# A reordered front with a third mask tile, and a sync queue that holds three loads for another one

## The chip, the cores and the metric

The program runs on one core of one Trainium2 chip. The metric is the device time of one execution in microseconds (us); lower is better. The core has a matrix engine (TensorE, PE in the profile, with its weight loads as PEld), a vector engine (DVE), a scalar engine (ACT), a general engine (GpSimd, POOL) and a sync engine (SP) that here only issues transfers. ACT and POOL issue a few transfers too. Rows ending in q (SPq, ACTq, POOLq) are the issuing side of such a transfer.

## What is computed

Two batches of 8 heads, 768 positions, head size 40: a gated recurrent attention, computed in chunks of 128 positions, then two feed-forward layers of width 1536 over the resulting 1536 x 320 matrix.

```python
for t in range(S):                                   # per batch and head
    m_new = max(f[t] + m, i[t])                      # stabiliser
    C = exp(f[t] + m - m_new) * C + exp(i[t] - m_new) * outer(v[t], k[t])
    n = exp(f[t] + m - m_new) * n + exp(i[t] - m_new) * k[t]
    y[t] = sigmoid(o[t]) * (C @ q[t]) / max(abs(n @ q[t]), 1)
x = (sigmoid(x @ w_gate) * (x @ w_val)) @ w_out      # first layer
x = ((x @ w_a) * (x @ w_b)) @ w2_out                 # second layer
```

## The kernel before

Every (batch, position block) pair is a chunk n, 12 in all; n % 2 is the batch. The first four chunks (0 to 3) are done alone, in a stretch called the front here. It ends when the first product of the feed-forward layer, `up(0, 0)` (line 580), starts. From there on TensorE runs `up` and `down` (line 597) units without a break, and the work of the chunks 4 to 11 is put between them. The order of each engine's work is written out by hand.

In a chunk, TensorE does four things. `spread` (line 440) multiplies a selection matrix with a tile `arow` (128 x 1024): its rows are a triangular mask except for rows 0 and 32, which receive the high and the low half of a running maximum (`a_hi`, `a_lo`) by transfers; the product lays that row out over 128 partitions, in PSUM. `scores` (line 477) multiplies keys `k` and queries `q_blk`, in two halves; a half needs both. `values` takes the state times scaled queries `q` (line 493; only from chunk 2 on) and then adds the weights `pt` times values `vk` (line 502). `to_state` (line 516) adds to the state and needs `v_w`. `turn` (line 528) transposes the finished rows, and `columns` (line 537) the gates.

ACT makes `pt` (`weigh`, line 687) from the spread rows; DVE multiplies it with the scores (`product`, line 893), zeroes one row of it (`dve_fix`, line 896), and divides the values (`combine`, lines 903 to 911). POOL weighs the values (`weigh_v`, 1099), multiplies with the output gate (`open_x`, 1109 and 1110), and scales the queries (`scale_q`, 1117), for which `load_scaled` on SP brings a copy of the queries (`q`, line 328) and a scale row repeated over 40 partitions (`i_rep`, line 333, three transfers). That scale row was made by ACT (`i_rows`, line 737) and goes through a scratch tensor in HBM (`i_scratch`, line 350).

Chunks use two sets of tiles in turn, so `arow[0]` serves the chunks 0, 2 and 4: the rows of chunk 2 are loaded only when `spread(0)` has read the tile (`pe_ab`). The keys and queries of chunk 3 come from POOL's own transfer queue (lines 1183 and 1186), with a semaphore of their own, `ld_q_own`, complete at 64. The other loads of the front go out from SP in written order, and a wait there holds everything behind it. Two layers' weights come as 24 tiles `w_raw` (line 346), split into `w_hi` and `w_lo`.

Of the kernel before, what the change touches and what calls it, by code (L numbers as in the profile page):

```python
# [19 lines left out]
F32 = mybir.dt.float32  # L20
# [7 lines left out]
P = 128  # L28
# [3 lines left out]
VW = HD + 1  # L32
# [32 lines left out]
def use_of(n):  # L65

    return n // 2 if n < ALONE else n - 2

# [23 lines left out]
def build(nc, f_in, i_in, q_in, kq3_in, vk_in, o_in, w1_in, w2_in, consts_in, bm_in, out):  # L92
    ctx = ExitStack()
    with ctx:
# [49 lines left out]
        both = [sb("k_both", [TRI, HEADS * P]), q_blk[0]]  # L144
        stack = [sb(f"{x}_stack", [TRI, HEADS * P], F32R) for x in "kq"]
# [35 lines left out]
        pool_q, pool_v, pool_d, pool_x = (sem(n) for n in ("pool_q", "pool_v", "pool_d", "pool_x"))  # L181
        ld_q_own, pool_wup = sem("ld_q_own"), sem("pool_wup")
# [88 lines left out]

        @block.sync
        def _(sp):
            def load_rows(n):

                s = set_of(n)
                if n > ALONE:
                    sp.wait_ge(act_e, 2 * n)
                else:
                    wait(sp, pe_ab, 2 * before(n) + 2)  # L280
                if n > ALONE:
                    sp.dma_start(levels[s][:, :],
                                 a_dram[n * HEADS * P:(n + 1) * HEADS * P].partition_broadcast(P)).then_inc(ld_a[s], 16)
                    return
                for at, tile in ((HI, a_hi), (LO, a_lo))[:1 if n < BATCH else 2]:
                    sp.dma_start(arow[s][at:at + 1, :].bitcast(F32), row_source(tile, n)).then_inc(ld_a[s], 16)  # L286
# [7 lines left out]
            def load_q(n):  # L294

                s = set_of(n)
                if n >= BATCH:
                    load_k(n)
                for j, k in ((0, 3), (1, 3), (2, 2)):
# [54 lines left out]
            load_k(0)  # L354
            load_k(1)
            sp.wait_ge(dve_zero, 1)
            load_q(0)
# [9 lines left out]
            load_v(1)  # L367
            sp.wait_ge(dve_split, 4)
# [60 lines left out]
        def _(pe):  # L429
            def spread(n):  # L430

                s = set_of(n)
                pe.wait_ge(ld_a[s], 32 * (use_of(n) + 1))
                for half in range(2):
                    if n < BATCH:
                        pass
                    else:
                        pe.wait_ge(act_e, (0, 4, 6)[n - 2] + half + 1)
                        wait(pe, act_cols, 4 if n == 2 and half == 0 else 0)
                    pe.matmul(spread_bank(n, half)[:, :], sel[:, :], arow[s][:, half * HALF:(half + 1) * HALF],  # L440
                              start=True, stop=True).then_inc(pe_ab, 1)
# [37 lines left out]

            def values(n):  # L480
# [15 lines left out]
                if n <= ALONE:  # L496
                    pe.wait_ge(dve_fix, n + 1)
# [108 lines left out]
            scores(0, 0)  # L606
            pe.wait_ge(ld_ident, 16)
# [66 lines left out]
        def _(act):  # L674
# [78 lines left out]
            def rows_out(group):  # L753

                for tb in (0, 2):
# [8 lines left out]
                    else:  # L764
# [12 lines left out]
                     tri_t[:, :].unsqueeze(1).to_broadcast([P, HEADS, P])).then_inc(tri_set1, 1)  # L777
            act.wait_ge(dve_split, 2)
# [15 lines left out]
            for c in range(2, CHUNKS):  # L794
                i_rows(c)
# [5 lines left out]
            x_high(0)  # L801
            x_high(1)
# [47 lines left out]
        def _(dve):  # L850
# [34 lines left out]
            def product(n, half):  # L885
# [8 lines left out]
                if half and n <= ALONE:  # L894
                    dve.wait_ge(dve_p, 2 * n + 2)
                    dve.memset(pt[s][LO:LO + 1, LO - 1::P], 0.0).then_inc(dve_fix, 1)
# [96 lines left out]
            dve.memset(q_blk[0][:, :], 0.0).then_inc(dve_zero, 1)  # L993
# [99 lines left out]
        def _(pool):  # L1093
# [34 lines left out]
            def mask(n):  # L1128

                level = levels[set_of(n)][:, :].rearrange("s (h t) -> s h t", t=P)  # L1130
                pool.wait_ge(ld_a[set_of(n)], 32 * (BATCH + 1) + 16 * (n - ALONE))
# [24 lines left out]
            for at in (HI, LO):  # L1156
# [12 lines left out]
                               channel_multiplier=-1).then_inc(pool_own, 1)  # L1169
            pool.wait_ge(act_cols, 2)  # L1170
            weigh_v(0)
            weigh_v(1)
# [9 lines left out]
            pool.wait_ge(pe_s, 4)  # L1182
            pool.dma_start(k3[1][:, :], kq3_in[3, :, 0:3 * P]).then_inc(ld_q_own, 16)
            for j, k in ((0, 3), (1, 3), (2, 2)):
                own = slice(j * HD, (j + 1) * HD)
                pool.dma_start(q_blk[1][own, 3 * j * P:(3 * j + k) * P],
                               kq3_in[3, own, 3 * P:(3 + k) * P]).then_inc(ld_q_own, 16)
# [85 lines left out]
```

## Time and profile before

| | us |
|---|---|
| median of 3 runs (lowest, highest) | 465.87 (465.13, 466.97) |
| the profiled execution, its own time | 466.42 |
| its span, first to last instruction | 464.7 |
| TensorE busy in the span | 457.4 |
| first `up` product starts | 35.02 |

The profiled execution's time is 1.7 us more than its span. The span is counted from the first instruction, and all positions below are us from there. After 35 us the chain that ended last consists of TensorE's units `up` and `down` and chunk work between them, one behind the other.

### The profile page before, as it was taken

How to read it: one execution, taken by the hardware profiler on the slowest of the kernel's cores; microseconds unless marked ns; L12 is line 12 of the kernel's file. 1: busy time of each engine (PE TensorE's matmuls, PEld its weight loads, DVE VectorE, ACT ScalarE, POOL GpSimd, SP SyncE). 2: the span in 40 equal slices, each digit the busy share in tenths (PEclk: the TensorE clock that was granted, in tenths of full speed). 3: DMA queues.
4: the chain of work that ended last, by engine and by line, in shares of the span. 5: the costliest groups of instructions: out<-in, count | busy, mean ns of one | idle time of the engine just before them, and what ended most of it. 6: DMA issues, size and time to landing. Idle time of an engine off the chain costs nothing.

```text
span 464.7 us, 6645 instructions
## 1 busy us (share of the span) xinstructions
PE 457.4 (98%) x2527; PEld 404.6 (87%) x2527; DVE 206.4 (44%) x365; ACT 197.2 (42%) x362; POOL 87.7 (19%) x99
## 2 busy tenths in 40 slices
PE   8989999999999999999999999999999999999996
PEld 5888899898889899888889889889988998898896
DVE  8858876766564644434132253222313222322322
ACT  5954949567382846234253352213222221312222
POOL 4573322303313020102454360000000000000000
PEclk9989999999999999999999999999999999999999
DMA  5878595542524460001322300000000000100001
GB/s 157 233 214 300 162 271 189 161 161 85 161 84 126 117 225 10 1 1 31 112 98 63 130 0 1 1 1 0 26 31 1 1 1 0 58 0 1 0 1 57
DMA packets 22005, 38.06 MB, mean 82 GB/s; under 512 B 2910, under 2 KB 16225, under 8 KB 21973
## 3 DMA queue, kind: packets, MB, share of 16 engines
q1 hardware_dynamic: 21605, 36.58, 25.7%
q10 hardware_dynamic: 208, 0.71, 0.5%
q8 instruction: 20, 0.33, 0.3%
q0 software_dynamic: 160, 0.35, 0.2%
q14 instruction: 12, 0.10, 0.1%
HBM read 35.55 MB, written 2.04 MB: 81 GB/s over the span
## 4 chain that ended last, share of the span: by engine, by line
PE 94%; DMA 2%; SPq 1%; POOL 1%; issue 1%; DVE 0%; POOLq 0%; DVEq 0%
PE bank L580 57%; PE bank L597 27%; PE bank L502 3%; PE bank L468 1%; PE bank L493 1%; PE bank L516 1%; PE bank L558 1%; PE bank L528 1%; DMA vk<-vk_in 1%; SPq L286 1%; DMA f_row<-f_in 1%; DMA i_scratch<-f_row 0%; PE bank L477 0%; POOL q L1117 0%; DMA arow<-a_lo 0%
## 5 line engine op out<-in xcount | busy, mean ns | idle before, releaser
L751 ACT CAST h_hi<-h_ff 128x512 fp32r<-128x512 f32 x72 | 44.6, 619 | 175.5 <-PE bank L597 95.2
L580 PE MATMUL bank<-xt,w_hi 128*128 128x512 f32 x360 | 117.9, 392 | 0.0
L968 DVE TENSOR_TENSOR h_lo<-h_ff,h_hi 128x512 fp32r<-128x512 f32 x72 | 52.8, 733 | 122.4 <-ACT h_hi L751 122.4
L962 DVE TENSOR_TENSOR h_ff<-bank,s_ff 128x512 f32<-128x512 f32 x72 | 49.8, 691 | 110.0 <-PE bank L580 106.0
L580 PE MATMUL bank<-xt,w_lo 128*128 128x512 f32 x216 | 84.3, 390 | 0.0
L580 PEld LDWEIGHTS bank<-xt,w_hi 128*128 128x128 f32 x360 | 66.2, 188 | 12.8 <-issue 0.2
L744 ACT ACTIVATE s_ff<-bank 128x512 f32<-128x512 f32 x72 | 43.0, 597 | 75.0 <-PE bank L580 74.1
L580 PE MATMUL bank<-xt,w_hi_end 128*128 128x512 f32 x180 | 58.8, 392 | 0.0
L580 PE MATMUL bank<-xt,w_hi_mid 128*128 128x512 f32 x180 | 58.8, 391 | 0.0
L580 PEld LDWEIGHTS bank<-xt,w_lo 128*128 128x128 f32 x216 | 40.5, 188 | 8.7
L597 PE MATMUL bank<-w_hi,h_hi 128*128 128x320 f32 x144 | 45.0, 313 | 0.0
L597 PE MATMUL bank<-w_lo,h_hi 128*128 128x320 f32 x144 | 44.4, 309 | 0.0
L597 PE MATMUL bank<-w_hi,h_lo 128*128 128x320 f32 x144 | 44.4, 308 | 0.0
L580 PE MATMUL bank<-xt,w_lo_end 128*128 128x512 f32 x108 | 42.2, 390 | 0.0
L580 PE MATMUL bank<-xt,w_lo_mid 128*128 128x512 f32 x108 | 42.2, 390 | 0.0
L580 PEld LDWEIGHTS bank<-xt,w_hi_mid 128*128 128x128 f32 x180 | 33.3, 188 | 6.4
L580 PEld LDWEIGHTS bank<-xt,w_hi_end 128*128 128x128 f32 x180 | 33.3, 188 | 6.4
L597 PEld LDWEIGHTS bank<-w_lo,h_hi 128*128 128x128 f32 x144 | 27.1, 188 | 0.7
L597 PEld LDWEIGHTS bank<-w_hi,h_hi 128*128 128x128 f32 x144 | 27.0, 188 | 0.6
L597 PEld LDWEIGHTS bank<-w_hi,h_lo 128*128 128x128 f32 x144 | 27.0, 188 | 0.0
L1139 POOL TENSOR_TENSOR w_lo<-w_raw,w_hi 128x1088 fp32r<-128x1088 f32 (+1 forms) x7 | 16.9, 2419 | 41.7 <-ACT w_hi L723 41.7
L580 PEld LDWEIGHTS bank<-xt,w_lo_end 128*128 128x128 f32 x108 | 20.3, 188 | 4.3
(128 smaller groups left out, 685.3 us busy)
## 6 DMA issues: line engine op xcount, KB each, us to landing
w_raw<-w_in SPq DMA_DIRECT2D x24, 544.0 KB, 4.0
vk<-vk_in SPq DMA_DIRECT2D x12, 344.0 KB, 3.2
levels<-a_scratch SPq DMA_DIRECT2D x7, 512.0 KB
k_both<-kq_in SPq DMA_DIRECT2D x21, 120.0 KB
q_blk<-kq_in SPq DMA_DIRECT2D x21, 120.0 KB
y<-rows_t SPq DMA_DIRECT2D x12, 160.0 KB, 1.9
q<-kq_in SPq DMA_DIRECT2D x10, 180.0 KB
osig_b<-o_in SPq DMA_DIRECT2D x8, 160.0 KB, 2.5
```

The source lines that it names most:

```text
L286: sp.dma_start(arow[s][at:at + 1, :].bitcast(F32), row_source(tile, n)).then_inc(ld_a[s], 16)
L468: mm = pe.matmul(st[:, h * P:(h + 1) * P], stack[0][:, own], stack[1][:, own], start=True, stop=True)
L493: mm = pe.matmul(acc[:, h * VW:(h + k) * VW], q3[s][:, x * P:(x + 1) * P], cst[p][:, h * VW:(h + k) * VW], start=(x == 0), stop=False)
L502: mm = pe.matmul(acc[:, h * VW:(h + 1) * VW], pt[s][:, h * P:(h + 1) * P], vk[s][:, h * VW:(h + 1) * VW], start=(n < BATCH and h == 0), st ...
L516: mm = pe.matmul(sc[0:TRI, h * VW:(h + k) * VW], vk[s][:, row:row + TRI], v_w[n % 2][:, h * VW:(h + k) * VW], start=True, stop=True)
L580: mm = pe.matmul(up_bank(u, gv)[:, :], w_part(low, f, (gv * 3 + kt) * P, P), xt[:, xb * TOK + g * TG:xb * TOK + (g + 1) * TG], start=(j == ...
L597: mm = pe.matmul(OB[tb][:, 0:DM], h[r][:, tb * P:(tb + 1) * P], w_part(low, f, W1C, DM), start=(f == 0 and j == 0), stop=(f == NF - 1 and ...
L744: act.activation(s_ff[u % 2][:, :], up_bank(u, 0)[:, :], ACT.Sigmoid if u < UNITS // 2 else ACT.Copy).then_inc(act_s, 1)
L751: act.copy(h_hi[u % 2][:, :], h_ff[u % 2][:, :]).then_inc(act_h, 1)
L962: dve.tensor_tensor(h_ff[u % 2][:, :], up_bank(u, 1)[:, :], s_ff[u % 2][:, :], ALU.mult).then_inc(dve_h, 1)
L968: dve.tensor_tensor(h_lo[u % 2][:, :], h_ff[u % 2][:, :], h_hi[u % 2][:, :].bitcast(F32), ALU.subtract).then_inc(dve_hlo, 1)
L1139: pool.tensor_tensor(w_part(1, j % NF, at, WC - at), w_raw[j % RING][:, at:], w_part(0, j % NF, at, WC - at).bitcast(F32), ALU.subtract).t ...
```

## The change

- A third mask tile `arow[2]` for chunk 2, laid over `k_stack`, which is first written later. ACT fills it with one more copy of the mask, and chunk 2's high row no longer waits for `spread(0)`. Its low row is loaded by POOL's queue.
- `scores(0, 1)` comes right after `scores(0, 0)`; `spread(1)` stands between the halves of `scores(1)`; `values(0)` is cut into two halves, with `spread(2)` between them; DVE zeroes the row of chunk 0 by halves.
- SP: queries of chunk 0 before the keys of chunk 1, `vk` of chunk 1 later, and the rows of chunk 3 before the scaled queries of chunk 2. Ahead of those stands a new wait, `ld_q_own` at 64. It holds the scaled queries of the chunks 2 and 3, `vk` of 2 and 3, and the first `w_raw`. The store `d_scratch` goes behind the scaled queries of chunk 3; queries 4 and `w_raw` 1 go ahead of the second `i_scratch` store.
- POOL: the keys and queries of chunk 3 are issued ahead of `weigh_v(1)` and five small operations.
- ACT: the four `i_rows` of the chunks 4 to 11 stand behind `x_high(0)` instead of ahead of the gate's sigmoid; the load of the gates `osig_a` is issued after `weigh(1, 0)` is complete.

```diff
+def arow_of(n):
+    return 2 if n == 2 else set_of(n)
...
-                    wait(sp, pe_ab, 2 * before(n) + 2)
+                    wait(sp, pe_ab, (0, 0, 0, 4, 2)[n])
...
             sp.dma_start(f_row[:, :], f_in).then_inc(ld_gate, 16)
             load_k(0)
+            load_q(0)
             load_k(1)
-            sp.wait_ge(dve_zero, 1)
-            load_q(0)
...
             load_v(0)
-            load_v(1)
-            sp.wait_ge(dve_split, 4)
+            sp.wait_ge(tri_set2, 1)
+            sp.wait_ge(dve_split, 3)
             load_rows(2)
             load_q(2)
             sp.wait_ge(act_irow, 1)
             store_rows(f_row, i_dram, 1, 2, st_irow)
-            sp.wait_ge(dve_zero, 3)
+            load_v(1)
+            sp.wait_ge(dve_split, 4)
+            load_rows(3)
+            sp.wait_ge(dve_zero, 5)
             sp.wait_ge(st_irow, 16)
+            sp.wait_ge(ld_q_own, 64)
             load_scaled(2)
-            load_rows(3)
+            load_v(2)
+            load_scaled(3)
             sp.wait_ge(dve_dec, 1)
             sp.dma_start(d_dram, d_row[:, :]).then_inc(st_dec, 16)
-            load_v(2)
-            load_scaled(3)
             load_v(3)
             load_w(0)
...
+            load_q(4)
+            load_w(1)
             sp.wait_ge(act_irow, CHUNKS - 1)
             store_rows(f_row, i_dram, 2, CHUNKS, st_irow)
-            load_q(4)
-            load_w(1)
...
             scores(0, 0)
+            scores(0, 1)
...
-            scores(0, 1)
             scores(1, 0)
+            spread(1)
             scores(1, 1)
-            spread(1)
+            values_of(0, 0)
             spread(2)
-            values(0)
+            values_of(0, 1)
             to_state(0)
...
+            act.copy(arow[2][:, :].rearrange("k (h t) -> k h t", t=P),
+                     tri_t[:, :].unsqueeze(1).to_broadcast([P, HEADS, P])).then_inc(tri_set2, 1)
...
             weigh(1, 0)
+            weigh(1, 1)
+            act.wait_ge(act_e, 3)
             act.dma_start(osig_a[:, :], o_in[:, 0:ALONE * DM]).then_inc(ld_oa, 16)
-            weigh(1, 1)
             act.wait_ge(act_cols, 3)
             weigh(2, 0)
             weigh(2, 1)
-            for c in range(2, CHUNKS):
-                i_rows(c)
...
             x_high(0)
+            for c in range(2, CHUNKS):
+                i_rows(c)
             x_high(1)
...
+            pool.wait_ge(tri_set2, 1)
+            pool.wait_ge(dve_split, 4)
+            pool.dma_start(arow[2][LO:LO + 1, :].bitcast(F32), row_source(a_lo, 2)).then_inc(ld_lo_two, 16)
             pool.wait_ge(act_cols, 2)
             weigh_v(0)
+            pool.wait_ge(pe_s, 4)
+            pool.dma_start(k3[1][:, :], kq3_in[3, :, 0:3 * P]).then_inc(ld_q_own, 16)
+            for j, k in BLOCKS:
+                own = slice(j * HD, (j + 1) * HD)
+                pool.dma_start(q_blk[1][own, 3 * j * P:(3 * j + k) * P],
+                               kq3_in[3, own, 3 * P:(3 + k) * P]).then_inc(ld_q_own, 16)
             weigh_v(1)
```

SP's queue before, from the scaled queries of chunk 2 (`q_0`) to the first weight tile:

```order
L328 DMA q_0<-kq_in 120x384 [waits st_irow,dve_zero]
L333 DMA i_rep<-i_scratch 40x3x128 x2
L333 DMA i_rep<-i_scratch 40x2x128
L286 DMA arow<-a_hi 1x8x128 [waits pe_ab]
L286 DMA arow<-a_lo 1x8x128
L378 DMA d_scratch<-d_row 16x6 [waits dve_dec]
L322 DMA vk<-vk_in 128x688 [waits pe_t,pe_fv]
L328 DMA q_1<-kq_in 120x384
L333 DMA i_rep<-i_scratch 40x3x128 x2
L333 DMA i_rep<-i_scratch 40x2x128
L322 DMA vk<-vk_in 128x688 [waits pe_t,pe_fv]
L346 DMA w_raw<-w_in 128x1088
```

The same place of SP's queue in the changed kernel, from the rows of chunk 3 on:

```order
L297 DMA arow<-a_hi 1x8x128 [waits pe_ab,dve_split]
L297 DMA arow<-a_lo 1x8x128
L342 DMA q_0<-kq_in 120x384 [waits ld_q_own,st_irow,dve_zero]
L347 DMA i_rep<-i_scratch 40x3x128 x2
L347 DMA i_rep<-i_scratch 40x2x128
L336 DMA vk<-vk_in 128x688 [waits pe_t,pe_fv]
L342 DMA q_1<-kq_in 120x384
L347 DMA i_rep<-i_scratch 40x3x128 x2
L347 DMA i_rep<-i_scratch 40x2x128
L396 DMA d_scratch<-d_row 16x6 [waits dve_dec]
L336 DMA vk<-vk_in 128x688 [waits pe_t,pe_fv]
L360 DMA w_raw<-w_in 128x1088
```

The rows of chunk 3 have gone ahead of the wait, the store `d_scratch` behind chunk 3's scaled queries, and `q_0` waits for `ld_q_own` besides.

ACT before, from the four `i_rows` (line 737) past the gate's sigmoid (line 797) to the first two `x_high` (line 221):

```order
L737 ACTIVATE f_row<-m_row,m_prev 16x128 [waits dve_gate] x4
L797 ACT_TABLE_LOAD
L797 ACTIVATE osig_a<-osig_a 128x1280 [waits ld_oa]
L687 ACT_TABLE_LOAD [waits pe_ab]
L687 ACTIVATE pt<-bank,g_col 128x128 [waits pe_fv]
L687 ACTIVATE pt<-bank,g_col 128x128 x3
L687 ACTIVATE pt<-bank,g_col 128x128 [waits pe_ab,pe_fv]
L687 ACTIVATE pt<-bank,g_col 128x128 x3
L730 COPY g_col<-bank 128x64 [waits pe_cols]
L731 ACTIVATE w_col<-bank 128x64
L221 CAST xt<-bank 128x3x128 [waits pe_r] x2
```

ACT in the changed kernel, from the sigmoid's table load to the second `x_high`:

```order
L830 ACT_TABLE_LOAD
L830 ACTIVATE osig_a<-osig_a 128x1280 [waits ld_oa]
L719 ACT_TABLE_LOAD [waits pe_ab]
L719 ACTIVATE pt<-bank,g_col 128x128 [waits pe_fv]
L719 ACTIVATE pt<-bank,g_col 128x128 x3
L719 ACTIVATE pt<-bank,g_col 128x128 [waits pe_ab,pe_fv]
L719 ACTIVATE pt<-bank,g_col 128x128 x3
L762 COPY g_col<-bank 128x64 [waits pe_cols]
L763 ACTIVATE w_col<-bank 128x64
L230 CAST xt<-bank 128x3x128 [waits pe_r]
L769 ACTIVATE f_row<-m_row,m_prev 16x128 [waits dve_gate] x4
L230 CAST xt<-bank 128x3x128 [waits pe_r]
```

The four `i_rows` have moved from ahead of the sigmoid to between the two `x_high`.

## Rows read from the trace of the kernel before

**Rows 1.** The page: the span, TensorE's busy time, the last-ending chain by engine.

```profile
span 464.7 us, 6645 instructions
PE 457.4 (98%) x2527; PEld 404.6 (87%) x2527; DVE 206.4 (44%) x365; ACT 197.2 (42%) x362; POOL 87.7 (19%) x99
...
PE 94%; DMA 2%; SPq 1%; POOL 1%; issue 1%; DVE 0%; POOLq 0%; DVEq 0%
```

**Rows 2.** Busy time by stretches of the front (first column), with clock and DMA.

```profile
core 0: us, PE busy (x) PEld busy (x) DVE busy (x) ACT busy (x) POOL busy (x), PEclk, DMA share, GB/s
...
24.00:27.00 3.00, 1.78 (x15) 1.53 (x15) 2.44 (x9) 0.48 (x1) 1.42 (x2) 1.00 0.43 77
27.00:30.00 3.00, 3.00 (x24) 2.91 (x23) 0.54 (x3) 1.28 (x2) 2.13 (x4) 0.87 0.83 259
30.00:33.00 3.00, 3.00 (x13) 2.46 (x13) 1.33 (x3) 1.99 (x7) 2.59 (x4) 0.56 0.68 175
```

**Rows 3.** TensorE's timeline: start, duration, instruction, idle time before and releaser.

```profile
8.28 2.86 PE L477 MATMUL bank<-q_blk,k 120*128 120x256 f32 x12
...
19.11 0.74 PE L440 MATMUL bank<-arow,sel 128*128 128x512 f32 x2 [0.49 <-DMA arow<-a_lo]
...
22.48 0.80 PE L493 MATMUL bank<-cst,q 120*128 120x123 f32 x6
...
26.72 0.87 PE L493 MATMUL bank<-cst,q 120*128 120x123 f32 x6 [1.22 <-POOL q L1117]
...
29.16 1.15 PE L440 MATMUL bank<-arow,sel 128*128 128x512 f32 x2
...
31.27 0.85 PE L528 MATMUL bank<-ident,x_n 128*128 128x128 f32 x3
...
35.02 0.69 PE L580 MATMUL bank<-xt,w_hi 128*128 128x512 f32 x2
```

**Rows 4.** POOL's timeline: chunk 3's keys and queries, and the two scalings.

```profile
12.33 0.73 POOL L1183 DMA_DIRECT2D k<-kq_in  x1
13.07 1.54 POOL L1186 DMA_DIRECT2D q_blk<-kq_in  x3
...
20.91 0.99 POOL L1117 TENSOR_TENSOR q<-q,i_rep 120x384 f32<-120x384 f32 x1
...
25.58 0.99 POOL L1117 TENSOR_TENSOR q<-q,i_rep 120x384 f32<-120x384 f32 x1 [1.88 <-DMA i_rep<-i_scratch]
```

**Rows 5.** SP's queue in order of time: start and issuing time.

```profile
13.53 0.33 SPq L328 DMA_DIRECT2D q<-kq_in  x1
13.90 1.59 SPq L333 DMA_DIRECT2D i_rep<-i_scratch  x3
...
18.70 1.13 SPq L333 DMA_DIRECT2D i_rep<-i_scratch  x3
```

**Rows 6.** Transfers, 20 to 22 us: a queue's packets, MB, share of 16 engines; an issue's landing.

```profile
q8 instruction: 1, 0.02, 8.6%
...
w_raw<-w_in SPq DMA_DIRECT2D x1, 544.0 KB, 7.7
```

**Rows 7.** Transfers issued in 12 to 16 us: the last of POOL's queue, us to landing.

```profile
q_blk<-kq_in POOLq DMA_DIRECT2D x1, 40.0 KB, 4.1
```

**Rows 8.** The chain that ended last, 11 to 21 us: start, time from issue to landing.

```profile
11.21 2.25 DMA i_scratch<-f_row
...
17.46 3.38 DMA vk<-vk_in
```

**Rows 9.** ACT's timeline: mask copy, `i_rows`, `weigh(3)`, third `x_high`.

```profile
3.60 1.04 ACT L776 CAST arow<-tri_t 128x1024 fp32r<-128x1024 f32 x1
...
15.89 1.26 ACT L737 ACTIVATE f_row<-m_row,m_prev 16x128 f32<-16x128 f32 x4
...
21.05 2.17 ACT L687 ACTIVATE pt<-bank,g_col 128x128 f32<-128x128 f32 x8
...
32.15 0.48 ACT L221 CAST xt<-bank 128x384 fp32r<-128x384 f32 x1 [1.00 <-PE bank L528]
```

More of the change, by code:

```diff
@@ L144, in build @@
         both = [sb("k_both", [TRI, HEADS * P]), q_blk[0]]
+        third = ExitStack()
+        arow = arow + (third.enter_context(nc.sbuf_tensor("arow2", [P, HEADS * P], F32R)),)
+        third.close()
         stack = [sb(f"{x}_stack", [TRI, HEADS * P], F32R) for x in "kq"]
@@ L269, in turn_of_rows @@
             return XY[1] if g == 0 else XY[tb % 2]
+        BLOCKS = ((0, 3), (1, 3), (2, 2))
         @block.sync
@@ L284, in load_rows @@
                     return
-                for at, tile in ((HI, a_hi), (LO, a_lo))[:1 if n < BATCH else 2]:
-                    sp.dma_start(arow[s][at:at + 1, :].bitcast(F32), row_source(tile, n)).then_inc(ld_a[s], 16)
+                for at, tile in ((HI, a_hi), (LO, a_lo))[:1 if n <= BATCH else 2]:
+                    sp.dma_start(arow[arow_of(n)][at:at + 1, :].bitcast(F32), row_source(tile, n)
+                                 ).then_inc(ld_a_two if n == BATCH else ld_a[s], 16)
             def load_k(n):
@@ L298, in load_q @@
                     load_k(n)
-                for j, k in ((0, 3), (1, 3), (2, 2)):
+                for j, k in BLOCKS:
+                    if n == 0:
+                        sp.wait_ge(dve_zero, j + 1)
                     own = slice(j * HD, (j + 1) * HD)
@@ L432, in spread @@
                 s = set_of(n)
-                pe.wait_ge(ld_a[s], 32 * (use_of(n) + 1))
+                if n == BATCH:
+                    pe.wait_ge(tri_set2, 1)
+                    pe.wait_ge(ld_a_two, 16)
+                    pe.wait_ge(ld_lo_two, 16)
+                else:
+                    pe.wait_ge(ld_a[s], (32, 32, 0, 64, 64)[n])
                 for half in range(2):
@@ L439, in spread @@
                         wait(pe, act_cols, 4 if n == 2 and half == 0 else 0)
-                    pe.matmul(spread_bank(n, half)[:, :], sel[:, :], arow[s][:, half * HALF:(half + 1) * HALF],
+                    pe.matmul(spread_bank(n, half)[:, :], sel[:, :], arow[arow_of(n)][:, half * HALF:(half + 1) * HALF],
                               start=True, stop=True).then_inc(pe_ab, 1)
@@ L478, in scores, with values_of @@
                 mm.then_inc(pe_s, 1)
+            def values_of(n, half):
+                pe.wait_ge(dve_fix, half + 1)
+                pe.wait_ge(ld_v[n], 16)
+                for h in range(half * HEADS // 2, (half + 1) * HEADS // 2):
+                    mm = pe.matmul(value_bank(n)[:, h * VW:(h + 1) * VW], pt[n][:, h * P:(h + 1) * P],
+                                   vk[n][:, h * VW:(h + 1) * VW], start=(h == 0), stop=(h == HEADS - 1))
+                if half:
+                    mm.then_inc(pe_fv, 1)
             def values(n):
@@ L496, in values @@
                 if n <= ALONE:
-                    pe.wait_ge(dve_fix, n + 1)
+                    pe.wait_ge(dve_fix, n + 2)
                 else:
@@ L893, in product @@
                 dve.tensor_tensor(pt[s][:, own], score_bank(n, half)[:, :], pt[s][:, own], ALU.mult).then_inc(dve_p, 1)
-                if half and n <= ALONE:
-                    dve.wait_ge(dve_p, 2 * n + 2)
-                    dve.memset(pt[s][LO:LO + 1, LO - 1::P], 0.0).then_inc(dve_fix, 1)
+                if n == 0 or half and n <= ALONE:
+                    dve.wait_ge(dve_p, 2 * n + half + 1)
+                    of = own if n == 0 else slice(0, 2 * HALF)
+                    dve.memset(pt[s][LO:LO + 1, of.start + LO - 1:of.stop:P], 0.0).then_inc(dve_fix, 1)
             def combine(n):
@@ L992, in _ @@
             dve.memset(h_hi[0][:, 0:P].bitcast(F32), 0.0).then_inc(dve_warm, 1)
-            dve.memset(q_blk[0][:, :], 0.0).then_inc(dve_zero, 1)
+            for j, k in BLOCKS:
+                dve.memset(q_blk[0][:, 3 * j * P:(3 * j + k) * P], 0.0).then_inc(dve_zero, 1)
             dve.memset(rst[:, 0:2 * P], 1.0).then_inc(dve_gate, 1)
@@ L1181, in _ @@
                                    base=(x + 2) * HD, channel_multiplier=-1).then_inc(pool_low, 1)
[L1182 to L1187, printed above, removed]
             open_x(0)
```

4 lines of the change are left out of this document (3 added, 1 removed).

## Prediction

> **What bounds the kernel now.** I read the page first: TensorE is busy for 457.4 of 464.7 us and makes up 94% of the chain that ended last [rows 1]. From the first `up` product at 35.02 us on it has no hole, and the change edits nothing behind that point but the order of a few loads and the four `i_rows`. So its worth is how much earlier `up(0, 0)` starts, less what is given back later.
>
> Next come the stretches of the front. Between 24 and 27 us TensorE is busy for only 1.78 of 3.00 us, and between 27 and 33 us it seems full, but at a granted clock of 0.87 and 0.56 [rows 2]: part of it at the lower level, 1.2 GHz instead of 2.4. The timeline names the hole. `values(3)` starts at 26.72 after 1.22 us of waiting for POOL's scaling [rows 3], and that scaling starts at 25.58 after 1.88 us of waiting for `i_rep` [rows 4]. The other hole is 0.49 us ahead of `spread(3)` at 19.11, which waits for a row load [rows 3].
>
> Why is `i_rep` of chunk 3 late? Its issue ends at 18.70 + 1.13 = 19.83 [rows 5], and it is used at 25.58, 5.7 us later. Other transfers take 2.25 and 3.38 us to land, counted from the start of their issue [rows 8]. So 2.3 to 3.4 us are beyond the usual. In that time one instruction packet holds 8.6% of 16 engines for 2 us, that is one engine for 0.086 x 16 x 2 = 2.75 us, and the weight tile behind it takes 7.7 us to land [rows 6]. My reading is that a transfer is complete only when its slowest engine is, and that one engine was taken by an instruction fetch. The fetch is not removed by this change.
>
> **The hold.** `ld_q_own` completes when the last of POOL's four transfers lands: issued at 13.07 + 2/3 of 1.54 = 14.1, landed 4.1 us later, at 18.2 [rows 4, 7]. In the changed kernel the five small operations are no longer ahead of them, so they start when the scores of chunk 1 are done, at 8.28 + 2.86 = 11.1 [rows 3] instead of 12.33; TensorE's work up to there is the same in amount. That makes 17.0; with less traffic beside it perhaps 16.5. I take 16.9.
>
> Behind the waiting instruction on SP stand the scaled queries of chunk 2 (3.4 us later than now, since `q` went out at 13.53), `vk` 2, the scaled queries of chunk 3, `d_scratch`, `vk` 3, `w_raw` 0, the rows of chunk 4 and all later loads. Issuing the scaled queries of chunk 2 takes 13.90 + 1.59 - 13.53 = 1.96 us [rows 5], so they are out at 18.9. With 2.3 to 3.4 us to land they are there at 21.2 to 22.3, and scaling takes 0.99 [rows 4]: ready at 22.2 to 23.3, where `values(2)` now starts at 22.48 [rows 3]. So this load, which has slack today, has none left. I take 22.6, nearer the lower end, because the load of keys that shared the engines has landed by then: +0.1 us.
>
> The scaled queries of chunk 3 need another 2.4 us of issuing, as from `vk` at 17.46 [rows 8] to 19.83 today (`vk`, `q` and `i_rep`, with the two rows and the store that stood ahead of them gone to other places): out at 21.3 against 19.83. They land at 23.6 to 24.7 by the usual time, and with all of the 2.75 us of the fetch on top at 26.3 to 27.4. Both ends are possible, since I can't see where in its program the fetch falls against the later transfers. I take a stall of about 1 us: landed 24.9, scaled 25.9, `values(3)` at 26.0 instead of 26.72. That is **-0.7 us**. TensorE itself is there in time: `values(2)` at 22.6, then 26.72 - 1.22 - 22.48 = 3.0 us for it and `turn(1)`, so 25.6.
>
> The Trainium skill, DMA: Bandwidth & Descriptors, Rules for kernel authors, advises to issue a transfer early and wait on its semaphore late, and so speaks against a hold that delays four loads to favour one. By it alone both scaled loads come later by what their issue is later, and only the rival of a slower kernel, below, would be left. The rows bear half of it out: the load of chunk 3 was issued 5.7 us ahead of its use and still came late, so early issue did not help it.
>
> **The clock.** From `values(3)` at 26.72 to `up(0, 0)` at 35.02 are 8.30 us. Inside, `spread(4)` takes 1.15 us where `spread(3)` takes 0.74, and from 29.16 to the end of `turn(2)` at 31.27 + 0.85 = 32.12 pass 2.96 us [rows 3]. At the ratio of 1.15 to 0.74 the same work at full clock takes 1.9 us, so a clock that stays up gives 1.1 us; behind `turn(2)` ACT's `x_high(2)`, the second half of `weigh(4)` and `x_high(3)` set the pace [rows 9], at any clock. In my case `values(3)` still waits 0.4 us where it now waits 1.22, after the same run of small products. Bounds: 0 and -1.1. I take the middle, **-0.55 us**.
>
> **ACT and the rest.** The four `i_rows` cost 1.26 us ahead of the sigmoid and of `weigh(3)` at 21.05 [rows 9]. Behind the change `weigh(3)` can start about 19.8, `open_x(0)` and DVE's products of chunk 3 with it. I cost this at nothing: `values(3)` waits for `i_rep`, not for `pt`, and `values(2)` for its own scaling. If the scaled queries came free, it would be what allows the early start. The `i_rows` now run while ACT waits for `turn(1)`; the second `i_scratch` store was issued later than this before too. The second mask copy on ACT takes 1.04 us like the first [rows 9] and stands ahead of ACT's own issue of the low rows of chunks 0 and 1; against it chunk 0's queries are issued and its scores done earlier. Reordering spreads, scores and the halves of `values(0)` moves waits, but leaves TensorE the same sum of work up to `spread(3)`, where it has waited for 0.49 us at most: I take 0, bounds -0.5 and +1.0. The third mask tile and the earlier rows of chunk 3 remove the 0.49 us ahead of `spread(3)`, which ends in the wait ahead of `values(2)`: 0 here. One more small memset on DVE is lost in this.
>
> **The sum.** -0.7 - 0.55 = -1.25 us. The profiled execution's own time, 466.42 us (span 464.7 and 1.7 around it), becomes 465.2; it lies 0.55 above the median of the three runs, so against the median of 465.87 I predict **464.6 us**. A difference below 0.5% (2.3 us) can't be told from no change for this kernel.
>
> **The rivals.**
>
> *Full gain (chance 0.27).* The fetch falls beside the critical transfer, chunk 3's scaled queries land at 23.6, and the clock stays up. `values(2)` at 22.3, `values(3)` right behind `turn(1)` at 25.3: -1.4, with -1.1 of clock and up to -0.5 of the early front: 463.4 down to 462.9. For it speaks that the fetch's 2.75 us is not seen to recur elsewhere in the front; against it that the fetch must come at about the same place of TensorE's program.
>
> *The hold makes it slower (0.20).* Both scaled loads land at their upper bounds: `values(2)` at 23.4 (+0.9), and chunk 3's at 27.4, scaled at 28.4, so `values(3)` at 28.5, +1.8 us, with the clock as now or worse: 467.7, up to 468.7 if it stays down for longer. It is one mechanism: SP waits till `ld_q_own`. It decides as soon as chunk 3's scaled queries land later than they do now, at 25.5; that needs an `ld_q_own` later than 17 together with the whole stall.
>
> *Nothing comes of it (0.08).* `up(0, 0)` starts earlier, but `values(4)` then waits for its own scaled queries, whose load now stands behind the later `i_scratch` store, and the gain is given back: 465.9.
>
> *My forecast* has 0.45, with its own range of 463.5 to 466.3.
>
> **How the numbers follow.** The range of 462.8 to 467.6 reaches from the full gain to the lower part of the slower rival and leaves out less than 2 in 10. Faster than 463.5 are most of the full gain and a bit of the forecast: 0.24. Slower than 468.2 is the end of the hold's rival: 0.08. Within 0.5%: 0.68.
>
> **What the profile after would show.** SP's `q` of chunk 2 at about 16.9 instead of 13.53; POOL's keys at 11.2; scaling of chunk 2 at 21.2 to 22.3 with a wait for `i_rep` that isn't there now; scaling of chunk 3 at about 24.9; `values(3)` at 26.0; `up(0, 0)` at 33.8; one instruction packet of over 1 us between 19 and 22. A granted clock of 1.00 through 27 to 33 us would show the full gain. I am wrong if `ld_q_own` completes well before 16 or after 18, or if behind 34 us a hole opens ahead of `values(4)`.

## The result: slower, and the profile after

The changed kernel takes **470.09 us** (median of 6 runs, 468.98 to 472.26), the kernel before beside it 465.32 us (6 runs, 464.28 to 466.97): a ratio of **1.0098, interval 1.0071 to 1.0125**. The profiled execution took 471.42 us with a span of 469.7. I had predicted 464.6, and at most 467.6. The ratios here and below leave disturbed runs out, which matters most for the one kernel of the experiments e5 and e12: without 4 of its 24 runs, at 471.8 to 472.3 us, its means are 1.5 and 2.0 us below the kernel before, with them 1.1 below and 0.1 above.

The page of the changed kernel, span, busy time, granted clock and last-ending chain; it answers to [rows 1]:

```profile
span 469.7 us, 6653 instructions
PE 462.3 (98%) x2527; PEld 409.3 (87%) x2527; DVE 206.9 (44%) x368; ACT 198.0 (42%) x363; POOL 89.8 (19%) x100
...
PEclk9968999999999999999999999999999999999999
...
PE 95%; DMA 1%; ACT 1%; issue 1%; POOL 0%; DVE 0%; POOLq 0%
```

TensorE has the same 2,527 products and is busy for 4.9 us more. So it didn't just wait longer: the same products took longer. The fourth slice (35.2 to 47.0 us) is still at 0.8, the third at 0.6. The stretches of the front show where it begins, beside [rows 2]:

```profile
21.00:24.00 3.00, 0.96 (x11) 0.70 (x10) 1.43 (x3) 2.99 (x14) 0.10 (x1) 1.00 0.43 98
24.00:27.00 3.00, 1.96 (x14) 1.99 (x14) 0.78 (x3) 0.90 (x4) 2.85 (x5) 0.82 0.94 283
27.00:30.00 3.00, 3.00 (x15) 3.00 (x16) 0.74 (x4) 0.17 (x1) 1.57 (x2) 0.50 0.78 250
...
36.00:39.00 3.00, 3.00 (x12) 2.39 (x12) 1.23 (x4) 1.71 (x6) 3.00 (x3) 0.50 0.55 157
39.00:42.00 3.00, 3.00 (x18) 2.64 (x17) 2.49 (x5) 2.46 (x3) 2.47 (x4) 0.90 1.01 379
```

From 21 to 24 us TensorE is busy for 0.96 of 3.00. Then the clock falls to 0.50, which is 1.2 GHz, and all four stretches from 27 to 39 stand at 0.50. Before, only parts of 27 to 33 were that low. Who makes the hole is in SP's waits and SP's queue, which answer to [rows 5] (the first two rows: us in total, times, longest):

```profile
SPq L391 <- DMA q_blk<-kq_in: 7.1, 1, 7.1
SPq L342 <- DMA i_scratch<-f_row: 4.0, 1, 4.0
```

```profile
18.93 0.34 SPq L342 DMA_DIRECT2D q<-kq_in  x1
19.30 2.63 SPq L347 DMA_DIRECT2D i_rep<-i_scratch  x3
22.03 0.36 SPq L336 DMA_DIRECT2D vk<-vk_in  x1
22.43 0.59 SPq L342 DMA_DIRECT2D q<-kq_in  x1
23.06 1.14 SPq L347 DMA_DIRECT2D i_rep<-i_scratch  x3
```

Line 391 is the hold. Chunk 2's scaled queries go out at 18.93 instead of 13.53, and issuing takes 2.63 us, not 1.59. POOL, beside [rows 4]: keys issued earlier, the first scaling at 23.90 instead of 20.91.

```profile
11.52 0.59 POOL L1213 DMA_DIRECT2D k<-kq_in  x1 [1.19 <-PE bank L498]
12.10 1.53 POOL L1216 DMA_DIRECT2D q_blk<-kq_in  x3
...
23.90 1.00 POOL L1154 TENSOR_TENSOR q<-q,i_rep 120x384 f32<-120x384 f32 x1 [2.94 <-DMA i_rep<-i_scratch]
```

TensorE, beside [rows 3]: `values(2)` (lines 524 and 533) and `values(3)`, and the first `up`.

```profile
25.04 0.87 PE L524 MATMUL bank<-cst,q 120*128 120x123 f32 x6 [3.08 <-POOL q L1154]
25.75 3.37 PE L533 MATMUL bank<-vk,pt 128*128 128x41 f32 x16
...
29.59 1.41 PE L524 MATMUL bank<-cst,q 120*128 120x123 f32 x6
30.80 3.55 PE L533 MATMUL bank<-vk,pt 128*128 128x41 f32 x16
...
40.87 0.69 PE L611 MATMUL bank<-xt,w_hi 128*128 128x512 f32 x2
```

`values(2)` starts 2.56 us later than before (22.48), and from there to `up(0, 0)` pass 15.83 us instead of 12.54: +3.29. Together `up(0, 0)` is 5.85 us late. From it to the end of the span pass 469.7 - 40.87 = 428.8 us; before, 464.7 - 35.02 = 429.7.

### The profile page after: what moved, and what is told of

It is laid out like the page before. It is cut to its first block, busy times and chain, and to the rows that moved or that the text cites. A ratio compares the mean times of both kernels' runs of the same rounds, so it can differ in the third digit from the quotient of the medians.

```text
span 469.7 us, 6653 instructions
## 1 busy us (share of the span) xinstructions
PE 462.3 (98%) x2527; PEld 409.3 (87%) x2527; DVE 206.9 (44%) x368; ACT 198.0 (42%) x363; POOL 89.8 (19%) x100
## 4 chain that ended last, share of the span: by engine, by line
PE 95%; DMA 1%; ACT 1%; issue 1%; POOL 0%; DVE 0%; POOLq 0%
PE bank L611 56%; PE bank L628 27%; PE bank L533 4%; PE bank L524 2%; DMA osig_a<-o_in 1%; PE bank L489 1%; PE bank L547 1%; PE bank L559 1%; PE bank L498 1%; PE bank L575 1%; PE bank L589 1%; ACT pt L719 1%; ACT osig_a L830 0%; POOL q L1154 0%; PE bank L461 0%
## 5 line engine op out<-in xcount | busy, mean ns | idle before, releaser
L1176 POOL TENSOR_TENSOR w_lo<-w_raw,w_hi 128x1088 fp32r<-128x1088 f32 (+1 forms) x7 | 16.9, 2417 | 41.7 <-ACT w_hi L755 41.7
L533 PE MATMUL bank<-vk,pt 128*128 128x41 f32 x176 | 24.1, 303 | 0.0
```

The source lines that it names most:

```text
L533: mm = pe.matmul(acc[:, h * VW:(h + 1) * VW], pt[s][:, h * P:(h + 1) * P], vk[s][:, h * VW:(h + 1) * VW], start=(n < BATCH and h == 0), st ...
L1176: pool.tensor_tensor(w_part(1, j % NF, at, WC - at), w_raw[j % RING][:, at:], w_part(0, j % NF, at, WC - at).bitcast(F32), ALU.subtract).t ...
```

## The experiments

Twelve experiments ran (eleven kernels, since e12 is e5 once more), in three groups of four, with 4 to 12 runs each beside 25 to 35 of the kernel before. The medians are over all of them. The last three columns are of one profiled run each, which isn't always a typical one (e1's took 468.32, e7's 470.61 and e11's 471.10 us, 2 to 4 above their medians): clock over the whole span, start of `up(0, 0)`, and what is left from there to the end.

| run | median us | ratio to before, interval | clock | up | up to end |
|---|---|---|---|---|---|
| before | 465.0 to 465.7 | 1 | | 35.02 | 429.7 |
| changed | 470.09 | 1.0098 [1.0071, 1.0125] | 0.985 | 40.87 | 428.8 |
| e1: changed, no hold | 466.31 | 1.0040 [1.0005, 1.0075] | 0.996 | 32.95 | 433.7 |
| e2: before, hold alone | 469.25 | 1.0069 [1.0042, 1.0097] | 0.988 | 38.37 | 429.6 |
| e3: changed, idle products | 469.94 | 1.0095 [1.0065, 1.0126] | 0.999 | 35.45 | 431.9 |
| e4: before, idle products | 465.99 | 1.0002 [0.9976, 1.0029] | 0.999 | 33.87 | 429.7 |
| e5: e1, scale rows back | 464.09 | 0.9982 [0.9963, 1.0001] | 1.0 | 32.79 | 429.1 |
| e6: changed, scale rows back | 468.12 | 1.0032 [0.9994, 1.0070] | 0.988 | 37.68 | 428.7 |
| e7: changed, hold one step later | 468.56 | 1.0074 [1.0040, 1.0108] | 0.985 | 40.03 | 428.9 |
| e8: before, scale rows late | 466.44 | 1.0030 [0.9999, 1.0062] | 1.0 | 33.03 | 431.6 |
| e9: e6, idle products | 466.52 | 1.0022 [0.9994, 1.0050] | 1.0 | 35.15 | 429.3 |
| e10: e5, gate load sooner | 464.39 | 0.9977 [0.9946, 1.0008] | 0.999 | 32.32 | 429.2 |
| e11: e2, idle products | 467.18 | 1.0030 [0.9993, 1.0067] | 1.0 | 37.64 | 431.8 |
| e12: e5 once more | 464.22 | 0.9950 [0.9920, 0.9981] | 1.0 | 33.26 | 428.8 |

Idle products write a bank that is free at the time and change no result. "Scale rows" are the four `i_rows` and the second `i_scratch` store. "Up to end" is the reading aid: near 429 the rest runs without a hole that costs; over 431 something is late behind the front, or the clock falls there.

### e1, the changed kernel without the hold

```diff
-            sp.wait_ge(ld_q_own, 64)
             load_scaled(2)
```

> The changed kernel without SP's wait for ld_q_own, all else as changed. Theory (the hold): the wait held the scaled queries of chunk 2 until 18.9 us and pushed values(2) from 22.48 to 25.04; without it they go out at about 12.3, values(2) starts at or before 22.0, the clock stays up for at least 10 us of the 13.7 us that it was low, and the time is that of the kernel before or 1 to 3 us less (462.5 to 465.5). Rival (the rest of the reordering, above all the slower landing of chunk 3's keys and of the gates): the time stays within 1.5 us of the changed kernel (468.5 to 471.5).

3.8 us come back in the median, but not all: 466.31 is above the theory's 462.5 to 465.5. In its profile the front is the best so far: `values(2)` at 22.81, `up(0, 0)` at 32.95, 2.07 us ahead of before. All of it and more is lost behind, at `turn(4)` (line 558), where the clock then falls too (0.68 from 45 to 48 us). Six of the ten runs kept 0.999 or more and took 465.3 to 466.3 us, so the fall isn't typical; but even these runs don't show the front's gain against the kernel before. TensorE's rows, then the second `i_scratch` store (line 364) and chunk 4's scaled queries in SP's queue:

```profile
32.95 0.70 PE L610 MATMUL bank<-xt,w_hi 128*128 128x512 f32 x2
...
46.11 0.90 PE L558 MATMUL bank<-ident,x_n 128*128 128x128 f32 x3 [2.19 <-POOL x_n L1146]
```

```profile
26.59 0.43 SPq L364 DMA_DIRECT2D i_scratch<-f_row  x1
31.18 0.33 SPq L342 DMA_DIRECT2D q<-kq_in  x1
...
41.50 0.35 SPq L293 DMA_DIRECT2D levels<-a_scratch  x1
```

Chunk 4's scaled queries go out at 31.18, where they went out at 29.09 before, and `levels` at 41.50 instead of 40.13. So I had a second suspect beside the hold.

### e2, the hold alone in the kernel before

```diff
-            load_scaled(2)
             load_rows(3)
+            sp.wait_ge(ld_q_own, 64)
+            load_scaled(2)
```

> The kernel before with two edits: chunk 3's rows are issued ahead of chunk 2's scaled queries, and then SP waits for ld_q_own at 64. Theory (the hold): SP resumes at 18.2 us instead of 13.5, chunk 2's scaled queries are ready at 23 to 24, values(2) starts 1.5 to 2.5 us later and the clock falls ahead of it: 468 to 471. Rival (the rest of the reordering): a wait of this kind is covered, 464 to 466.5.

The hold alone makes the kernel before 0.69% slower. The profile has two small holes, 0.88 us ahead of `values(2)` at 23.06 (for the scaling) and 0.94 ahead of `values(3)` at 26.97 (for DVE's `x_raw`). Then the clock is at 0.50 from 27 to 36 us. So `values(2)` need be only 0.6 us later than in [rows 3] to lose 3.35 us up to `up(0, 0)`.

```profile
23.06 0.87 PE L494 MATMUL bank<-cst,q 120*128 120x123 f32 x6 [0.88 <-POOL q L1118]
...
26.97 1.54 PE L494 MATMUL bank<-cst,q 120*128 120x123 f32 x6 [0.94 <-DVE x_raw L912]
```

Of its ten runs one kept a clock of 0.999, and that one took 464.85 us; the others had 0.984 to 0.989 and took 468.7 us or more.

### e3 and e4, idle products that fill the hole

```diff
             turn(0)
+            turn_over(13)
             values(2)
```

> The changed kernel with 13 idle products of 128x512 (about 2.8 us at full clock, zeros into a free bank) in TensorE's hole ahead of values(2); no result depends on them. Theory (the hold costs 2.6 us of start and the low clock the rest): values(2) starts at 25.0 to 25.3 as now, but the low clock between 26 and 39.6 is gone or shrinks to one stretch of 3.4 us, and the time falls by 3 to 5 us, to 465 to 467. Rival (the clock doesn't matter, as much of this work is small products that wait for each other): the time stays at 469.5 to 471.

A miss in the time (465 to 467 was expected) that told most. The mechanism is right: with TensorE kept busy for 3.25 us in the hole, the clock stays at 1.00 and `up(0, 0)` starts at 35.45 instead of 40.87. From `values(2)` at 25.75 the same work takes 9.70 us, not 15.83: **the low clock costs 5 to 6 us of the front**. (The idle products overshoot the hole: POOL's scaling, which `values(2)` waits for, ended at 23.31 in this run, 2.4 us before it starts.) Yet the time is the same. The gain is lost at the same place as in e1:

```profile
35.45 0.70 PE L611 MATMUL bank<-xt,w_hi 128*128 128x512 f32 x2
...
48.20 0.55 PE L559 MATMUL bank<-ident,x_n 128*128 128x128 f32 x3 [1.79 <-POOL x_n L1148]
```

e4 puts five such products into the kernel before, ahead of `values(3)`.

```diff
             turn(1)
+            pe.wait_ge(act_cols, 6)
+            for _ in range(5):
+                pe.matmul(bank[2][:, :], ...)
             values(3)
```

> The kernel before with 5 idle products of 128x512 (about 1.1 us) in the hole of 1.2 us ahead of values(3). Theory (a hole tips the clock): the stretch at half clock from 29.2 to 32.6 us goes away, up(0, 0) starts 1.1 us earlier, 464.2. Rival (the clock falls because values(2) and values(3) are many small products, hole or not): no change, 465.3, within 0.5.

In the profile `up(0, 0)` is 1.15 us earlier than before, with no late hole, as the theory had it, but the median is the same, not 464.2. Most of the kernel before's other runs have a clock of 0.997 or more (16 of the 25 beside e4): its clock is seldom down for long, so there was little to win.

### e5 and e6, the scale rows back in their places

```diff
             weigh(2, 1)
+            for c in range(2, CHUNKS):
+                i_rows(c)
             act.wait_ge(ld_oa, 16)
...
             x_high(0)
-            for c in range(2, CHUNKS):
-                i_rows(c)
...
-            load_q(4)
-            load_w(1)
             sp.wait_ge(act_irow, CHUNKS - 1)
             store_rows(f_row, i_dram, 2, CHUNKS, st_irow)
+            load_q(4)
+            load_w(1)
```

> The changed kernel without the hold, and with the four i_rows of the chunks 4 to 11 back ahead of the gate's sigmoid and the second i_scratch store back ahead of queries 4 and w_raw 1. Theory A (late supply: without the hold, the front's gain of 2.07 us, up at 32.95 instead of 35.02, was lost because the second i_scratch store and all loads behind it came late): the hole of 2.2 us ahead of turn(4) at about 44 us is gone or under 0.5, TensorE keeps full clock behind it, and from up to the end it takes about 430 instead of 433.6 us; time 463 to 464. Theory B (the hole comes from something else that the reordering delays, such as osig_a's gate load or the weight tiles): time stays at 466 to 466.5 and the hole stays.

> The changed kernel with the hold kept, and only i_rows and the second i_scratch store back where they were. Theory A (the hold costs by the hole ahead of values(2) and the fall of the clock, which keeps TensorE late enough for the late loads to be hidden): no difference from the changed kernel, 469.5 to 470.5, up at 40 to 41, half clock for over 10 us. Theory B (the later scale rows are a cost of their own, in addition to the hold): 1 to 2 us less than the changed kernel, 468 to 469.

e5 is as theory A has it: chunk 4's scaled queries go out at 27.51 instead of 31.18, there is no wait left on TensorE from 36 to 52 us, and 429.1 us remain behind `up(0, 0)`. With the hold and the later scale rows undone, what is left of the reordering is no loss. The edit moves the `i_rows` on ACT and the store on SP together; which of the two counts was not separated.

e6 missed theory A. With the hold kept, the same edit brings 2 us, as theory B said (the intervals of its ratio, 0.9994 to 1.0070, and the changed kernel's just don't overlap); yet its profile shows little of it (up at 37.68, since `values(2)` happened to start at 23.34). The single runs explain it: of 12, the 4 with a clock of 0.996 or more took 464.2 to 465.7, and the 8 at 0.985 to 0.992 took 467.9 to 471.3. It looks as if the hole ahead of `values(2)` were at the edge where the clock sometimes stays; the runs without a profile don't show how long their hole was. Where it stays, the late scale rows decide: the one run of the changed kernel at 0.996 still took 468.98, and e3 at 0.996 to 1.000 took 469.1 to 471.3.

### e7, the hold one step later

```diff
-            sp.wait_ge(ld_q_own, 64)
             load_scaled(2)
+            sp.wait_ge(ld_q_own, 64)
             load_v(2)
```

> The changed kernel with the hold one step later: SP issues the scaled queries of chunk 2 first, then waits for ld_q_own, then vk of 2 and the scaled queries of chunk 3. Theory A (the loss is the late scaled queries of chunk 2): values(2) starts at 22.5 to 23 instead of 25.04, values(3) at 26 to 27.5, the half clock lasts under 5 us, time 465.5 to 467. Theory B (the loss is that vk, the scaled queries of chunk 3 and the loads behind them are late, whichever load is held): values(3) still after 28.5, half clock for over 8 us, time 469 to 470.

Chunk 2's scaled queries are there in time, and it is slow all the same, 468.56. TensorE and DVE in the profiled run:

```profile
19.76 1.89 PE L498 MATMUL bank<-q_blk,k 120*128 120x384 f32 x8
23.19 0.42 PE L568 MATMUL bank<-ident,i_row 16*128 16x16 f32 x4 [1.54 <-DVE x_raw L947]
...
24.17 1.27 PE L524 MATMUL bank<-cst,q 120*128 120x123 f32 x6
```

```profile
19.83 0.86 DVE L1065 TENSOR_TENSOR a_lo<-m_row,a_hi 16x128 fp32r<-16x128 f32 x1
20.62 1.48 DVE L1067 TENSOR_TENSOR s_row<-i_row,m_row 16x512 f32<-16x512 f32 x1
...
22.65 0.49 DVE L947 TENSOR_TENSOR x_raw<-bank,rec 128x320 f32<-128x320 f32 x1
```

TensorE waits for DVE, which finishes `combine(1)` behind `a_lo` and `s_row`. The two took 0.86 and 1.48 us here, where they took 0.28 and 0.67 in the changed kernel, and DVE waited for no transfer. So nothing shows that the hold made this hole. In e5 TensorE waited 1.46 us too, but *ahead of* the scores of chunk 3, and kept its clock. Here it waited 1.54 behind them, with only small products to follow, and the clock fell at 24 us and was at 0.50 from 27 to 36. So a hole from another source can cost the clock too, not only that of the late scaled queries.

But this run, at 470.61, is one of the slowest three of eight, and only two of them have a clock of 0.985. The two runs that kept 0.999 or more took 468.42 and 467.55 us, still 1 to 3 us over e1's runs at such a clock (465.3 to 466.3). So neither theory fits: the median lies between the two ranges, and what the hold costs here with the clock up isn't shown; the transfers that it still holds (`vk` of 2 and 3, the scaled queries of chunk 3) are the candidates.

### e8, the scale rows late in the kernel before

The edit of e5 and e6 in reverse, on the kernel before.

> The kernel before with only the i_rows of the chunks 4 to 11 moved behind the first x_high, and queries 4 and w_raw 1 ahead of the second i_scratch store. Theory A (late scale rows cost behind the front): up stays at about 35, a hole of 1 to 2 us opens ahead of values(4) or turn(4) at 40 to 48, time 467 to 468. Theory B (they are hidden, as I predicted): within 0.3% of the kernel before, 465 to 467, no new hole.

In its profile `up(0, 0)` starts 2 us earlier than before (the scaled queries of chunk 3 came in time in this run), and 431.6 us remain behind it; SP waited 5.0 us for the store's landing, where it waits 1.7 in the kernel before. The hole ahead of `turn(4)` is only 0.37 us long, though; with it TensorE's waits from 35 to 100 us come to 1.2 us (the longest, 0.6, for DVE's `xt`), where the kernel before has none. They don't prove the late scale rows: e11, which has these rows in their old places, waits for the same three producers and for as long. The interval of the ratio, 1.0030, just touches 1.

### e9, both mended, the hold still there

e6's edit and e3's idle products together.

> The changed kernel with its hold, the i_rows and the second i_scratch store back in their old places, and 13 idle products of TensorE (into a bank that is read by nobody then; they change no result) ahead of values(2), in the hole that the hold makes. Theory A (the loss has two parts that cover for one another: the low clock that follows the hole, and the late scale rows; only with both mended is the time back): up at 34.5 to 36, clock 0.996 to 1.00 in nearly all runs, no hole over 1 us from 40 to 48 us; time 464.5 to 466, so a ratio of 1.000 within 0.003. Theory B (the hold costs by itself, by loads that come late, whatever the clock does): time 467 to 469, with TensorE waiting for weight tiles or POOL behind 36 us.

The decisive experiment. Either edit alone leaves the changed kernel at 468.1 or 469.9; both together bring it to 466.52, 3.6 us of the 4.8 back, with the hold in place. That is 0.5 us above theory A's range and as far below theory B's, but the clock (0.996 or more in all 12 runs), the start of `up(0, 0)` and the missing hole are A's:

```profile
21.62 3.23 PE L575 MATMUL bank<-h_hi 128*128 128x512 f32 x13
24.69 0.80 PE L524 MATMUL bank<-cst,q 120*128 120x123 f32 x6
25.32 1.92 PE L533 MATMUL bank<-vk,pt 128*128 128x41 f32 x16
```

```profile
27.00:30.00 3.00, 3.00 (x29) 3.00 (x29) 1.65 (x6) 1.38 (x2) 1.88 (x3) 1.00 0.85 281
```

```profile
35.15 0.70 PE L611 MATMUL bank<-xt,w_hi 128*128 128x512 f32 x2
...
46.03 0.55 PE L559 MATMUL bank<-ident,x_n 128*128 128x128 f32 x3 [0.21 <-POOL x_n L1148]
```

`values(2)` starts at 24.69, nearly as late as in the changed kernel (25.04), and the same 16 products take 1.92 us instead of 3.37. e9 is still 2.3 us above e12, the same kernel without hold and idle products. Part of that can be the idle products' own time, as POOL's scaling had ended at 24.11: e6's four runs that kept the clock without them took 464.2 to 465.7 us. How much isn't shown.

### e10, e11, e12

```diff
             weigh(1, 0)
+            act.dma_start(osig_a[:, :], o_in[:, 0:ALONE * DM]).then_inc(ld_oa, 16)
             weigh(1, 1)
-            act.wait_ge(act_e, 3)
-            act.dma_start(osig_a[:, :], o_in[:, 0:ALONE * DM]).then_inc(ld_oa, 16)
```

> The changed kernel without the hold, with i_rows and store back as in the run of that kind before, and the load of the gates osig_a issued ahead of weigh(1, 1) again, without its wait. Theory A (osig_a's load shares the transfer engines with chunk 3's keys and delays both, which is why scores(3) waited 1.46 us for q_blk): the wait ahead of scores(3) is under 0.8 us, up at 32 to 32.6, time 463.3 to 464. Theory B (the keys are late by their own issue and the rest of the traffic, osig_a does not matter, and behind the front the loads are the bound): 464 to 464.5, same as without this edit, or slower if the sigmoid's chain is not what matters.

The wait ahead of the scores of chunk 3 is gone. Rows of e5, of e12 (the same kernel) and of e10:

```profile
20.16 2.00 PE L497 MATMUL bank<-q_blk,k 120*128 120x384 f32 x8 [1.46 <-DMA q_blk<-kq_in]
```

```profile
19.83 2.00 PE L497 MATMUL bank<-q_blk,k 120*128 120x384 f32 x8 [0.81 <-DMA q_blk<-kq_in]
```

```profile
19.20 1.90 PE L497 MATMUL bank<-q_blk,k 120*128 120x384 f32 x8
```

The load of `osig_a` went out at 10.58 instead of 11.39 and 11.69, and the last part of chunk 3's queries landed 5.4 us after its issue instead of 7.0 and 6.4. `up(0, 0)` starts at 32.32, the earliest of all, but the median is that of e5 and e12: half a microsecond of front is less than these medians can tell.

> The kernel before with the hold alone (rows of chunk 3 ahead, then the wait for ld_q_own ahead of chunk 2's scaled queries), and idle products in both holes: 4 ahead of values(2), 5 behind turn(1) ahead of values(3). They change no result. Theory A (what the hold costs in this kernel is the clock: 10 us at the lower level for two holes of 0.9 us): clock 0.996 to 1.00, up at 34 to 35, time 465 to 466.5 instead of 469.25. Theory B (the late loads behind the hold cost 3 us by themselves): 468 to 469 with a full clock.

e11 puts 4 idle products ahead of `values(2)` and e4's five ahead of `values(3)` into e2. Of e2's 0.69% over before, 0.30% is left, with an interval from -0.07% to 0.67%, and the clock is 0.996 or more in all 12 runs. By these ratios over half of the hold's price in this kernel is the clock. Where the rest comes from, if it is real, stays open: the loads behind the hold (in its profile `values(2)` waits 0.83 us for `vk`) or the idle products' own time, for which e2's one run with the clock kept speaks (464.85, no slower than before). Its profiled run had POOL's keys over 2 us late (14.52, against 12.33), so its positions aren't compared.

> The changed kernel without the hold and with i_rows and the second i_scratch store in their old places once more, beside the other three, to narrow its interval. If it is the better version: ratio below 1 with the upper end of the interval below 1, 463.5 to 464.5. If the first result was luck: within 0.1% of the kernel before.

464.22 against 465.16. e5 and e12 are one kernel, with 0.9982 [0.9963, 1.0001] and 0.9950 [0.9920, 0.9981]: its ratios lie 0.2 and 0.5% below the kernel before, the first with an interval that just includes 1. It is clearly faster than the changed kernel; over the kernel before the gain is small, and the means given with the result leave it open.

## Why the prediction was wrong

**The bound held.** The change acts on the front and on `up(0, 0)`'s start; behind it the changed kernel needs 428.8 us, before 429.7. In the terms of my sum, `values(3)` came at 29.59 instead of 26.72, +2.87 us where I had -0.7, and from there to `up(0, 0)` passed 11.28 us instead of 8.30, +2.98 where I had -0.55.

**The hold: right place, wrong size.** I took `ld_q_own` at 16.9, with "less traffic beside it perhaps 16.5". It completed at about 18.85, which was one of my signs of being wrong ("after 18"). POOL's keys left at 11.52, close to the forecast 11.1, but the last part landed 5.7 us after its issue, not 4.1. The release is 2 us later than the term had it, and the issue of `i_rep` took 1.0 us longer. So `values(2)` came at 25.04 instead of 22.6, beyond the rival's 23.4. I overlooked two neighbours. `osig_a`, 640 KB, issued at 11.42, is now 0.1 us ahead of the keys, where it was 0.9 ahead, and took 7.0 us to land instead of 4.3. And `vk` of chunk 1, which the change itself moved: it goes out at 9.79, where both `vk` had gone out by 7.43, and lands at 13.5, beside the keys. Issues of the changed kernel from its view of 10 to 16 us: KB, us to landing:

```profile
osig_a<-o_in ACTq DMA_DIRECT2D x1, 640.0 KB, 7.0
vk<-vk_in SPq DMA_DIRECT2D x1, 344.0 KB, 3.7
...
q_blk<-kq_in POOLq DMA_DIRECT2D x1, 40.0 KB, 5.7
```

e10 has the last part land sooner with `osig_a` issued earlier. In e2, where `vk` is early and `osig_a` 0.5 us ahead of the keys, the last part landed in 3.6 us. No run moves `vk` of chunk 1 alone, so the shares of the two aren't shown. On the other side `values(3)` did lose its wait for `i_rep`, as I said; but my reading of that wait, an instruction fetch on one transfer engine, was tested by no run (the changed kernel has a packet of this kind too, 4.8% of 16 engines from 20 to 22 us, where before it was 8.6%).

**The clock: the step that failed.** I wrote "Bounds: 0 and -1.1" and took -0.55. That assumed that an edit could only shorten the low stretch of [rows 2]. The runs show +2.98 us behind `values(3)`, and +3.29 from `values(2)` to `up(0, 0)`, in which the wait of 1.22 has even gone; e3 and e9 put the price of the low clock in this work at 5.4 to 6.1 us (15.83 against 10.46 and 9.70). It decided the result more than the late start did: in e9 `values(2)` is 2.2 us later than before, and with the clock up `up(0, 0)` is only 0.13 us later (35.15). The right reading was there: the front of before already had its clock at 0.56 from 30 to 33 us, after 1.2 us of hole ahead of small products. A change that puts a wait ahead of such products has a loss to bound, not only a gain. e2 shows how steep it is: `values(2)` 0.6 us later, `up(0, 0)` 3.35 later. My rival of a slower kernel had the mechanism, but priced it by the wait alone, with "up to 468.7 if it stays down for longer".

**ACT and the rest: the second step that failed.** I costed the moved `i_rows` at nothing, since "the second `i_scratch` store was issued later than this before too". The store is issued 1.7 us later in e1 than before (26.59, 24.93), and at 29.47 in the changed kernel. There SP waits 4.0 us for its landing instead of 1.7: the landing takes about as long (4.5 and 4.1 us), but before the change SP issued queries 4 and `w_raw` 1 in that time. Chunk 4's scaled queries, `osig_b` and `levels` stand behind it. The rival "nothing comes of it" had this chain. It costs little as long as the low clock hides it (e6's runs at 0.985 took 469.8 to 471.3 us, the changed kernel's 470.1 to 471.4), which is why the profile of the changed kernel alone can't show it, and 2.2 and 3.4 us in the medians when the front is fast: e1 against e5, e3 against e9. In the kernel before it is 1.4 us, not clear of noise (e8). I also had `weigh(3)` start at about 19.8 once the `i_rows` were out of the way. It started at 21.05, as before, because the sigmoid ahead of it waited for `osig_a` till 18.46.

**Put together** (ratios over before, 1.0098 for the changed kernel): without the hold 1.0040, without the late rows 1.0032, without both 0.9982 and 0.9950. The two causes together are 1.2 to 1.5%, and what is left of the reordering is 0.2 to 0.5% below the kernel before, in those ratios. My forecast of -1.25 us (0.3%) falls in that range, but that is luck: it was made for the kernel with the hold, by terms that came out otherwise.

**Early issue.** The Trainium skill, DMA: Bandwidth & Descriptors, Rules for kernel authors, advises to issue a transfer early and to wait for it late. I had set that aside because one early issue had not helped. The runs agree with the page: the hold costs 0.58% of the changed kernel (against e1) and 0.69% of the kernel before (e2). One step later it is 0.34% (e7 against e1), which is not clear of noise.

**Open:** what e7, e9 and e11 still cost with the clock up, and the waits that e8 and e11 share behind `up(0, 0)`; and why the keys took 1.6 us longer to land, beside `osig_a` and `vk` of chunk 1. The total load wasn't the limit at the end: in the changed kernel the 16 transfer engines are busy for 0.28 of 16 to 17 us and 0.14 of 17 to 18, while the last part is still under way.

## What to carry to other kernels

Before adding a wait, look at the granted clock around the place where it will surface: if small products follow a hole there, bound the loss by the work behind it at half clock (here 5 to 6 us, in a stretch that takes about 10 at full clock), not by the hole. An experiment that mends one cause and changes nothing doesn't clear that cause: of two delays that hide each other, as here, the second may show only when both are mended. Moving a producer "into idle time" moves every transfer that stands behind its store in the queue.

## What the hardware showed unexpectedly

- Equal holes, unequal prices: 1.46 us ahead of the wide scores (e5) left the clock at 1.00; 1.54 us behind them, ahead of small products (e7), was followed by over 13 us at 0.50 (0.56 over 24 to 27, 0.50 to 36, 0.67 over 36 to 39). It is one profile each, and the holes differ in position too, so that the products behind them decide is my reading, not shown.
- In the changed kernel TensorE worked without a pause from 27 to 39 us (busy for 3.00 of every 3.00), and the clock stayed at 0.50 all that time. Most of it is the small products of `values`, `to_state` and `turn`, but wide ones too: `spread(4)` (128x512, at 34.14) and half the scores of chunk 4 (120x384, at 36.94). The first stretch above 0.50 is 39 to 42 us.
- 13 idle products in a hole of 3 us (e3) bought back 5.4 us of front.
